# Two gather buffers instead of six, and a looped VectorE stream, in the last expert stage of an attention and mixture-of-experts kernel

## The reference

```python
x = transpose(_attn_ref(q, k, v, w_phi))          # N = 2304 rows, D = 512
x = _moe_ref(x, w_gate, w1, w2)                   # dense: 8 experts on every row, Sinkhorn weights
return _moe2_ref(x, expert_emb, tau, w1, w2)      # each row goes to one expert only

def _moe2_ref(x, expert_emb, tau, w1, w2):
    logits = normalised(x) @ normalised(expert_emb).T / tau
    expert_idx = argmax(logits, axis=1); gate_w = softmax(logits)[row, expert_idx]
    for e in range(8):
        mask = expert_idx == e
        h = maximum(x[mask] @ w1[e], 0.0)         # 512 -> 1024
        out[mask] = gate_w[mask, None] * (h @ w2[e])   # 1024 -> 512
```

## Time and profile before

| | before |
|---|---|
| median of 3 runs | 2219.8 us (2208.98 to 2220.18) |
| the profiled execution | 2220.18 us |
| its span, first to last instruction | 2218.5 us |
| mean granted TensorE clock | 0.976 of full |
| PE busy | 2119.1 us, 96% |
| DVE, ACT, POOL busy | 982.2, 684.1, 131.8 us |
| chain that ended last, by engine | PE 91%, DVE 5%, issue 2%, ACT 1% |
| routed stage (L728 and L743 on the chain) | 8% and 6% |

### The profile page before, as it was taken

The page is one execution under the profiler, slowest core; times in us unless marked ns, Lnnn a source line. Parts: engine busy times, 40 slices in busy tenths (PEclk is TensorE's granted clock), DMA queues, the critical chain, the costliest instruction groups (busy, mean ns, idle before and its releaser), DMA issues.

```text
span 2218.5 us, 34602 instructions
## 1 busy us (share of the span) xinstructions
PE 2119.1 (96%) x13112; PEld 1272.6 (57%) x13113; DVE 982.2 (44%) x1565; ACT 684.1 (31%) x1351; POOL 131.8 (6%) x163
## 2 busy tenths in 40 slices
PE   5999899999999999999999999999999993999998
PEld 4888765555555555555555555555555563666665
DVE  5787845544454443444443444444444224222221
ACT  3555522333232332233332333332232220121211
POOL 0122220000000000000000000000000001111110
PEclk9999989999999999999999999999999985999999
DMA  6322011122122113212212211231222217211500
GB/s 183 89 61 64 22 39 38 39 77 85 68 77 76 39 39 114 77 39 77 78 44 109 76 39 39 77 114 39 76 77 76 105 48 303 105 40 71 214 10 7
DMA packets 93080, 169.03 MB, mean 76 GB/s; under 512 B 60438, under 2 KB 60566, under 8 KB 89760
## 3 DMA queue, kind: packets, MB, share of 16 engines
q1 hardware_dynamic: 88960, 157.92, 20.3%
q0 software_dynamic: 4000, 9.45, 1.2%
HBM read 126.19 MB, written 44.83 MB: 77 GB/s over the span
## 4 chain that ended last, share of the span: by engine, by line
PE 91%; DVE 5%; issue 2%; ACT 1%; POOL 0%; DMA 0%; DVEq 0%; POOLq 0%
PE ps L618 34%; PE ps L601 34%; PE ps L728 8%; PE ps L743 6%; PE ps L546 3%; PE ps L525 2%; PE ps L559 2%; DVE arena L955 1%; DVE fm L948 1%; PE ps L638 1%; PE ps L710 1%; PE ps L514 0%; DVE vm L1043 0%; PE ps L534 0%; DMA arena<-x_rows,rti 0%
## 5 line engine op out<-in xcount | busy, mean ns | idle before, releaser
L601 PE MATMUL ps<-arena 128*128 128x384 f16 x4608 | 774.7, 327 | 0.4 <-issue 0.4
L618 PE MATMUL ps<-arena 128*128 128x512 f16 x3456 | 773.4, 380 | 0.0
L601 PEld LDWEIGHTS ps<-arena 128*128 128x128 f16 x4608 | 451.5, 98 | 315.1 <-issue 3.4
L618 PEld LDWEIGHTS ps<-arena 128*128 128x128 f16 x3456 | 339.4, 98 | 395.0 <-issue 5.4
L842 ACT ACTIVATE arena<-ps 128x384 f32<-128x384 f32 x384 | 188.5, 491 | 1030.6 <-PE ps L601 1018.6
L1084 DVE TENSOR_TENSOR arena<-arena 128x384 f16<-128x384 f32 x384 | 214.3, 558 | 328.2 <-ACT arena L846 327.3
L1139 DVE SCALAR_TENSOR_TENSOR arena<-ps,wt,arena 128x512 f32<-128x512 f32 x126 | 94.6, 751 | 459.0 <-PE ps L618 459.0
L728 PE MATMUL ps<-arena 128*128 128x128 f16 x2400 | 180.9, 223 | 8.6 <-DVE arena L1329 8.3
L846 ACT ACTIVATE arena<-ps 128x384 f16<-128x384 f32 x384 | 186.0, 484 | 0.0
L728 PEld LDWEIGHTS ps<-arena 128*128 x2400 | 156.7, 98 | 37.6 <-issue 10.0
L1013 DVE SCALAR_TENSOR_TENSOR arena<-arena,wsc 128x1024 f16<-128x1024 f32 x128 | 164.2, 1285 | 6.2 <-ACT arena L811 6.1
(11 more groups left out here) (185 smaller groups left out, 1020.6 us busy)
## 6 DMA issues: line engine op xcount, KB each, us to landing
arena<-in_moe_w_dram SPq DMA_DIRECT2D x32, 2048.0 KB, 9.0
split_weights<-arena SPq DMA_DIRECT2D x16, 2048.0 KB, 7.4
arena<-split_weights SPq DMA_DIRECT2D x8, 4096.0 KB, 12.9
arena<-in_q_dram SPq DMA_DIRECT2D x16, 288.0 KB, 3.4
arena<-in_k_dram SPq DMA_DIRECT2D x16, 288.0 KB, 3.9
arena<-in_v_dram SPq DMA_DIRECT2D x1, 4608.0 KB, 16.0
x_rows<-arena SPq DMA_DIRECT2D x18, 256.0 KB, 3.8
arena<-in_v_dram SPq DMA_DIRECT2D x32, 128.0 KB, 2.3
```

What stands on the lines that cost most here:

```text
L601: last = pe.matmul(o, ring[:, slot, sw, FF * c + 128 * j:FF * c + 128 * j + 128], xT[:, sx, c, BLK * blk:BLK * blk + BLK], start=(n == 0), ...
L618: last = pe.matmul(ps[:, Y_PS + tt, :], hbuf[:, blk % 2, sh, f, 128 * tt:128 * tt + 128], ring[:, slot, 2 + sw, D * f:D * f + D], start=(n ...
```

## The change

The gather ring `xg` gets 2 slots instead of 6, so there are two semaphores `xg_in` instead of six, and POOL zeroes two slots instead of six. POOL's order becomes: gathers of tiles 0 and 1 ahead; then per step s gather(s+2), wait for rows_out(s), scatter(s). gather(s+2) waits until scale_rows(s) has read the slot. DVE's 25 steps are run by the same hardware loop as PE's and ACT's, so that column indices and some semaphore values come from registers within it. The scratch `R` of the routing stretch moves from the hidden-buffer area to the space behind `yo`.

```diff
-XB = 6
-        xg = take(XB * D).rearrange("p (u d) -> p u d", u=XB)
+        xg = take(2 * D).rearrange("p (u d) -> p u d", u=2)
...
+        R = take(10 * NT * E).rearrange("p (a n) -> p a n", a=10)
         at = [O_H]
...
-        R = take(10 * NT * E).rearrange("p (a n) -> p a n", a=10)
...
             def gather(s):
-                if due(s - XB + 1):
-                    pool.wait_ge(xs_done, s - XB + 1)
-                pool.indirect_dma_start(xg[:, s % XB, :], ...).then_inc(xg_in[s % XB], 16)
-            for s in range(XB - 1):
-                gather(s)
+                if due(s - 1):
+                    pool.wait_ge(xs_done, s - 1)
+                pool.indirect_dma_start(xg[:, s % 2, :], ...).then_inc(xg_in[s % 2], 16)
+            gather(0)
+            gather(1)
             for s in range(MT):
-                if s + XB - 1 < MT:
-                    gather(s + XB - 1)
+                if s + 2 < MT:
+                    gather(s + 2)
                 pool.wait_ge(yo_done, s + 1)
                 pool.indirect_dma_start(out, ...).then_inc(out_done[s % 2], 16)
...
-            for s in range(MT):
-                step2(s, s % 2)
+            tiles2(dve, step2, True)
```

More of the change, by code:

```diff
@@ L181, in pair_of @@
             return [sem(name + "0"), sem(name + "1")]
-        qk_in, v_in = pair_of("qk_in"), pair_of("v_in")
-        xg_in = [sem("xg_in" + str(n)) for n in range(XB)]
+        qk_in, v_in, xg_in = pair_of("qk_in"), pair_of("v_in"), pair_of("xg_in")
         vall_in, small_in, raw_in, w2_in = sem("vall_in"), sem("small_in"), sem("raw_in"), sem("w2_in")
@@ L285, in pairs, with tiles2 @@
             body(PAIRS // 2 - 1, False, True)
-        def tiles2(eng, step):
+        def tiles2(eng, step, counted=False):
             step(0, 0)
@@ L292, in tiles2 @@
                 for u in range(2):
-                    step(2 * c + u, u)
+                    step(2 * c + u, u, c) if counted else step(2 * c + u, u)
             for s in range(2 * (MT // 2 - 1), MT):
@@ L470, in _ @@
             pool.wait_ge(y_done, BT * NB * E)
-            for u in range(XB):
+            for u in range(2):
                 c(pool.memset(xg[:, u, :], 0.0))
@@ L476, in gather @@
             def gather(s):
-                if due(s - XB + 1):
-                    pool.wait_ge(xs_done, s - XB + 1)
-                pool.indirect_dma_start(xg[:, s % XB, :], None, x1_dram, bass.IndirectOffsetOnAxis(ap=rti[:, 0, s:s + 1], axis=0),
-                                        bounds_check=N - 1, oob_is_err=False).then_inc(xg_in[s % XB], 16)
-            for s in range(XB - 1):
-                gather(s)
+                if due(s - 1):
+                    pool.wait_ge(xs_done, s - 1)
+                pool.indirect_dma_start(xg[:, s % 2, :], None, x1_dram, bass.IndirectOffsetOnAxis(ap=rti[:, 0, s:s + 1], axis=0),
+                                        bounds_check=N - 1, oob_is_err=False).then_inc(xg_in[s % 2], 16)
+            gather(0)
+            gather(1)
             for s in range(MT):
-                if s + XB - 1 < MT:
-                    gather(s + XB - 1)
+                if s + 2 < MT:
+                    gather(s + 2)
                 pool.wait_ge(yo_done, s + 1)
@@ L1318, in col, with scale_rows @@
             def col(n, s):
-                return rt[:, n, s:s + 1]
-            def scale_rows(s, u):
-                dve.wait_ge(xg_in[s % XB], 16 * (s // XB + 1))
+                return rt[:, n, s:s + 1] if isinstance(s, int) else rt[:, n, bass.ds(s, 1)]
+            def scale_rows(s, u, count):
+                dve.wait_ge(xg_in[u], 16 * count)
                 if due(s - 1):
                     dve.wait_ge(xtr_done, s - 1)
-                dve.tensor_scalar(xs[:, u, :], xg[:, s % XB, :], col(5, s), None, ALU.mult).then_inc(xs_done, 1)
+                dve.tensor_scalar(xs[:, u, :], xg[:, u, :], col(5, s), None, ALU.mult).then_inc(xs_done, 1)
             def x_lo(s, u):
@@ L1343, in rows_out, with step2 @@
                 dve.tensor_scalar(yo[:, u, :], ps[:, 5 + u, :], col(6, s), None, ALU.mult).then_inc(yo_done, 1)
[L1345 to L1348, removed]
+            def step2(s, u, c=0):
+                more1 = not isinstance(s, int) or s + 1 < MT
+                more2 = not isinstance(s, int) or s + 2 < MT
+                n = s // 2 + 1 if isinstance(s, int) else c + 1
+                if more2:
+                    scale_rows(s + 2, u, n + 1)
+                if more1:
                     h_lo(s + 1, 1 - u)
-                if s + 2 < MT:
+                if more2:
                     x_lo(s + 2, u)
-                rows_out(s, u, s // 2 + 1)
-            scale_rows(0, 0)
-            scale_rows(1, 1)
+                rows_out(s, u, n)
+            scale_rows(0, 0, 1)
+            scale_rows(1, 1, 1)
             x_lo(0, 0)
```

## The result

The changed kernel takes 2252.8 us, the median of 4 runs (2250.98 to 2258.47), against 2216.9 us for the kernel before (4 runs). The ratio is 1.0169, with a 95% interval of 1.0147 to 1.0191: slower by 36 us between the medians, 37.5 by the ratio. The forecast was 2261 us, in a range of 2241 to 2275. Direction and range held; the loss is 3 to 5 us smaller than the forecast sum of 40.6, which still lies inside the interval (33 to 42 us).

What follows compares the result with a forecast made beforehand. The prediction took PE to bound the kernel, with 91% of the chain. Gathers beside loads 28.9, quiet steps 3.7 and clock 8.0 made 40.6 us on 2220.2, so 2261 us, in a range of 2241 to 2275.

Steps and rivals of the forecast that it cites:

- The path: Routed step: rows_out, scatter, gather, scale_rows, turn2 become one path; a gather landing within 3.7 us stays hidden.
- Four gathers beside a load: Routed steps where a gather meets a 4 MB weight load: PE waits before turn2, 28.9 us together.
- Rival C: Beside a load, queues get equal shares of bytes: stalls about 1.3 us each, clock holds; 2229 us, chance 0.04.
- The clock: PE's granted clock falls to half in all four long stalls, 2.0 us more each, 8.0 us.
- Rival A: PE's clock holds through the four stalls, as dense work came just before; 2253 us, chance 0.12.
- Quiet steps: Fifteen gathers of filled tiles without a load: lateness plus 0.3 us per step for DVE registers, 3.7 us.
- Rival B: DVE's loop adds 1 us to each step instead of 0.3; 2272 us, chance 0.09.
- The start: Second gather of the routed stage, 9.04 us on the chain: no gain expected, at most 4.8 us.
- Rival D: A gather issued alone passes a load in 3.5 us; 4.8 us gained at the start, 3.7 lost; 2219 us, chance 0.03.
- The sum: Whole kernel: gathers beside loads, quiet steps and clock together add 40.6 us to 2220.2, giving 2261 us.
- Everything before 1860 us unchanged: Sign expected in the changed profile: the part ahead of the routed stage stays as it was.

Runs made afterwards that it cites:

- the longer filler: The changed kernel with 38 matmuls into an unused bank added on PE ahead of turn2 of tile 3, where another run added 28; one run, 2255.6 us.
- its second profile: The kernel before, unchanged, profiled again to see whether the second gather of the routed stage lands late every time; one run, 2217.4 us.

## Why the prediction was right, and where its sizes were off

- *The path.* Right in each part: DVE, scatter, gather, scale_rows, turn2, with nothing behind turn2 late. No PE wait for x_lo or h_lo came up in the steps.
- *Four gathers beside a load.* Forecast 8.3, 6.4, 7.1 and 7.1 us, 28.9 together; measured 7.05, 7.11, 7.71 and 7.19, 29.1. The sum is closer than its terms, and that is luck: the first one's gather took 10.4 us here instead of the 11.5 of the earlier trace rows, and the other three waits were 0.1 to 0.7 us longer than forecast. Two of the rows that the forecast used, the 10.1 and 10.3 us of the earlier trace rows, belong to gathers of tiles 17 and 18, which hold few rows: the queue of scatters and gathers moved 0.19 and 0.18 MB around them, against 0.51 MB around the one of the earlier trace rows. They were a fair price all the same, because beside a load the landing hardly depends on the rows moved: without a load the same two tiles took 2.4 and 2.3 us in the changed kernel, and tiles 14 to 16, with 0.33 to 0.44 MB moved, took 10.2 to 10.5 beside one. Rival C, equal turns, would have given waits of 1.3 us and fails on all four.
- *The clock.* Forecast 8.0, 2.0 for each stall; it fell in all four. output2 took 7.46, 6.73, 7.58 and 6.50 us, so 1.2 to 2.2 more each and 6.9 together, and the transposes 0.5 more each; the gap of about 0.4 us behind turn2 went, so the four steps came out 35.6 us longer against a forecast of 36.9. That the fall is a cost of its own, and the idling's, is shown for the first of the four by the longer filler. Rival A is out.
- *Quiet steps.* Forecast 3.7 us over fifteen; all steps without a load together grew by 2.3. The 0.3 us per step for registers was right (0.31 in the step shown). Two of the fifteen gathers, those of tiles 17 and 18, landed after 2.4 and 2.3 us; before, they had been among the slow ones beside a load, and I had counted them as full. Rival B is out.
- *The start.* This is the term that was mis-sized: "I expect no gain; at most it falls to the 4.2 us of the first, 4.8 us gained." It fell to 3.6 us, and the stretch gained 4.5 us against the first profile of before. My reason was that gathers behind it in the same queue could not hold it up. With the load beside it, they can. The bound of 4.8 held, the choice of nothing did not. Rival D had this part right and its main part wrong.
- *The sum.* In the steps 35.6 + 2.3 = 37.9 us, against 40.6. With the 4.5 us gained at the start this is 33.4 us against the first profile of before, and 36.4 against its second, where the start gains 1.5. The timed runs say 36 to 37.5. That most timed runs of before start more like its second profile would explain it, but no run shows it.
- *Everything before 1860 us unchanged.* It was 3.2 us shorter, by the clock at the end of the dense stage, in code that the change leaves as it was.

## What to carry to other kernels

The depth of a prefetch is the place at which it is issued, not the number of its buffers; look in the order of the issuing queue for the step that needs it, and check that lead against the slowest landing in the trace, not the median. A transfer that shows no wait may be hiding a landing three times the usual one, and the load and the gather, which the end of the same output2 releases, met at all four loads in every profile in which neither was held back. A wait of PE cost its length here, and about 2 us more where the clock fell.

## What the runs showed of the hardware that I had not expected

The clock of TensorE fell behind idle times of 2.46 and 2.76 us that stood between dense matmuls, each time within about 0.6 us of the moment when PE began again, and stayed down for over 3 us; behind waits of 1.23 us and less it stayed up. Ahead of the stage's second hidden2 PE is idle for 2.13 to 2.18 us in all eleven profiles: the clock fell near the end of it in nine of them, and stayed at 1.00 in the two of the unchanged kernel before. Behind the four long waits it fell while PE was still idle. Idling is not the only thing that goes ahead of a fall: at the end of the dense stage of before it fell at 1801 and at 1814 us, while PE was on transposes and matmuls of 8 columns without a pause.

A gather behind its scatter took 3.1 to 3.5 us in quiet steps of the two kernels compared (2.3 and 2.4 for the tiles with few rows), and 10.0 to 11.9 with a 4 MB load issued 3 us earlier, in every profile in which the two met. The four loads themselves took 12.1 to 14.6 us. A gather that met the last part of a load took 6.4. The gather is done about when the load is, and that holds for gathers with few rows too: 10.1 us beside a load, 2.4 without, for the same tile.

Code that no experiment touched took up to 11 us more or less from profile to profile before the routed stage, and in the two compared here the granted clock in the last part of the dense stage differed, 0.85 against 1.00.
